# Preparing q and k for two attention heads at once, with DMAs that assemble each head's operands

## Chip, cores and metric

The kernel runs on one core of one Trainium2 chip. The metric is the device time of one execution in microseconds. A profiled execution has a span (first to last instruction) and a time of its own beside it.

## What is computed

Three stages, all on one core in one launch. Only the first is changed.

```
bits     = (x @ proj > 0) for x = q and x = k      # 6 bits a row: the bucket
mask     = q_bucket == k_bucket                     # per (batch, head)
scores   = where(mask, q @ k.T / 8, -1e9)           # 768 x 768
attn     = softmax(scores);  out = attn @ v         # 2 batches x 8 heads, head_dim 64
x        = out as (1536, 512)
y        = relu(x @ w_in)**2 @ w_out                # 512 -> 2048 -> 512
routed layer: tokens given to 8 experts by capacity, relu(y @ w1[e]) @ w2[e]
```

All values are fp32. A row of queries with no key in its bucket attends to all keys alike; this is the "fallback", made from the sum of v.

## The kernel before

`attention` handles the 16 heads one after another. TensorE, VectorE, ScalarE, GpSimd and SP (which issues the DMAs) each have a program written out in order, and they meet at semaphores. Four double PSUM banks are used: `PREP`, `ST`, `SM`, `O`. Tiles with a suffix 0 or 1 alternate by head (`i`, and `o = 1 - i` for the next head, `m = n + 1`).

While head `n` is attended to, head `n + 1` is prepared. Per head:

- `load` brings k and q (192 KB each, L148, L149), `load_v` brings v (L152), beside a half of ones in `v_raw`, so that one matmul yields numerators on 64 partitions and denominators on the other 64.
- `twice` on GpSimd (L194, L195) writes each row of q and k twice side by side; `transpose` (L476, `t_k`, `t_q`) turns them by six matmuls of 128 columns each, which gives both copies of the head on the two halves of the partitions.
- `k_high`, `q_high` (L256, L263) round to fp32r, `k_low`, `q_low` (L378, L383) subtract for the residual, `k_again`, `q_again` copy the high part again to where the scores need it. A high and a low part stand in the two halves of `ka` and `qa`, `qb`.
- `z_k`, `z_q` (L494, L495) project onto `proj`, with four matmuls of 384 columns each; `k_bits`, `q_bits` on VectorE and ScalarE turn signs into rows of 0, +-1 and 2^33 that stand below the high parts, so that a pair with unlike bits gets a hugely negative score from the same matmul.
- `scores` (L528) makes the scores row by row (two matmuls of 384 columns, six times), only for the row maxima, `row_max` (L400). `max_done`, then `rows` on TensorE (L537, L538) and ScalarE (L279, L280) bring the maxima and the sum of v into the operands of the next head (`qb`, `vsh`, and `vsl` for the residual, `v_low`, L414).
- `scores_t` (L515, L516) makes the transposed scores into the single bank `ST` (four matmuls of 384 columns, six times), `expo` (L285) the exponentials, `fallback` (L548) four matmuls, `weighted` (L552) multiplies with v: 12 calls of 384 columns in fp32, each two records in the profile.
- `numerator` (L421), `denominator` (L291), `invert` (L427: four reciprocals of 192 elements), `divide` and `low` on GpSimd (L212, L218) and `high` (L297) finish the head on its own 64 partitions, during the next one.

The order on TensorE of the steps of one head is written out by hand in `head` (L557). The last head's division is left to the beginning of `first_layer`. `load_weights` (L1389 to L1391) loads 8 MB for that stage once v of head 15 is issued; `first_layer` waits for it on `w_ready`. Between the stages all engines meet.

Of the kernel before, what the change touches and what calls it, by code (L numbers as in the profile page):

```python
# [6 lines left out]
BITS = 6  # L7
HEADS = B * NH
P = 128
# [3 lines left out]
PAIRS = HEADS // 2  # L13
TOK = B * S
# [15 lines left out]
FROW = D  # L30
MROW = 96
KF = MROW + 2
# [37 lines left out]
def attention(nc, banks, ident, finish, xt_hi, xt_lo, load_weights, q, k, v, proj):  # L70

    with ExitStack() as ctx:
# [3 lines left out]
        def sem(name):  # L82
            return ctx.enter_context(nc.semaphore("att_" + name))

        num, den, rden, xo = finish
        identr = sb("identr", [P, P], f32r)
        proj_sb = sb("proj_sb", [P, BITS])
        p_hh = sb("proj_hh", [P, P], f32r)
        p_ll = sb("proj_ll", [P, P], f32r)
        p_hl = sb("proj_hl", [P, P], f32r)  # L90
        p_h0 = sb("proj_h0", [P, P], f32r)
        off_q = sb("off_q", [P, 1])
        off_k = sb("off_k", [P, 1])
        guard = sb("guard", [P, 1])
        q_raw = [sb(f"q_raw{i}", [P, TT, D]) for i in range(2)]
        k_raw = [sb(f"k_raw{i}", [P, TT, D]) for i in range(2)]
        q_dup = sb("q_dup", [P, TT, 2, D])
        k_dup = sb("k_dup", [P, TT, 2, D])
        v_raw = [sb(f"v_raw{i}", [P, TT, P]) for i in range(2)]
        qa = [sb(f"qa{i}", [P, S], f32r) for i in range(2)]  # L100
        qb = [sb(f"qb{i}", [P, S], f32r) for i in range(2)]
        qc = [sb(f"qc{i}", [P, S], f32r) for i in range(2)]
        ka = [sb(f"ka{i}", [P, S], f32r) for i in range(2)]
        kb = [sb(f"kb{i}", [P, S], f32r) for i in range(2)]
        kg = sb("k_bits", [P, S])
# [3 lines left out]
        mn = sb("mn", [P, TT, KF], f32r)  # L109
# [3 lines left out]
        sel = sb("sel", [P, KF])  # L113
        vsh = [sb(f"vsh{i}", [P, P], f32r) for i in range(2)]
        vsl = [sb(f"vsl{i}", [P, P], f32r) for i in range(2)]
        PREP, ST, SM, O = banks

        names = ("zeroed", "made", "proj_in", "proj_split", "dup", "pool_steps", "tq", "tk", "zq", "zk", "st", "sm", "pv",
                 "mr", "qa_", "ka_", "qc_", "kc_", "qcs", "kbs", "ex", "mrc", "den_", "num_", "rec", "nrm", "xh", "xl",
                 "qlow", "klow", "fq", "fk", "mxs", "mns", "vslow", "vsum", "qk_in0", "qk_in1", "v_in0", "v_in1")  # L120
        (zeroed, made, proj_in, proj_split, dup, pool_steps, tq, tk, zq, zk, st, sm, pv,
         mr, qa_, ka_, qc_, kc_, qcs, kbs, ex, mrc, den_, num_, rec, nrm, xh, xl,
         qlow, klow, fq, fk, mxs, mns, vslow, vsum, qk_in0, qk_in1, v_in0, v_in1) = (sem(n) for n in names)
        qk_in, v_in = (qk_in0, qk_in1), (v_in0, v_in1)
# [5 lines left out]
        LOW, HIGH, BITROWS, TAIL = slice(0, D), slice(D, P), slice(FROW, FROW + FEAT), slice(MROW, KF)  # L130
# [7 lines left out]


        block = ctx.enter_context(nc.Block())  # L140

        @block.sync
        def _(sp):
            sp.dma_start(proj_sb[0:D, :], proj).then_inc(proj_in, 16)
            sp.dma_start(proj_sb[D:P, :], proj).then_inc(proj_in, 16)

            def load(n, i):
                sp.dma_start(k_raw[i][:], k_v[n]).then_inc(qk_in[i], 16)  # L148
                sp.dma_start(q_raw[i][:], q_v[n]).then_inc(qk_in[i], 16)  # L149

            def load_v(n, i):
                sp.dma_start(v_raw[i][:, :, VSL[i]], v_v[n]).then_inc(v_in[i], 16)  # L152
            load(0, 0)
            load(1, 1)
# [12 lines left out]
        @block.gpsimd  # L167
        def _(pool):
            pool.memset(ident[:], 0.0)
            pool.memset(sel[:], 0.0)  # L170
            pool.memset(off_q[:], 1.0)
            pool.memset(off_k[:], 1.0)
            pool.memset(guard[:], GUARD)
            pool.drain()
            pool.affine_select(out=ident[:], in_=ident[:], compare_op=ALU.not_equal, fill=1.0, base=0,
                               pattern=[[-1, P]], channel_multiplier=1)
            pool.memset(sel[:, KF - 1:KF], 1.0)
            pool.affine_select(out=off_q[:], in_=off_q[:], compare_op=ALU.is_ge, fill=0.0, base=-(FROW + BITS),
                               pattern=[[0, 1]], channel_multiplier=1)
            pool.affine_select(out=off_k[:], in_=off_k[:], compare_op=ALU.is_ge, fill=0.0, base=FROW + BITS - 1,  # L180
                               pattern=[[0, 1]], channel_multiplier=-1)
            pool.drain().then_inc(made, 1)

            def twice(m, i, count):

                pool.drain()
                pool.wait_ge(qk_in[i], count)
                if past(m, 1):  # L190
                    pool.wait_ge(tk, m)
                    pool.wait_ge(tq, m)
                pool.sem_inc(pool_steps, 1)
                pool.tensor_copy(k_dup[:], k_raw[i][:].unsqueeze(2).broadcast_to([P, TT, 2, D]))  # L194
                pool.tensor_copy(q_dup[:], q_raw[i][:].unsqueeze(2).broadcast_to([P, TT, 2, D])).then_inc(dup, 1)  # L195

            def sum_v(m, i, count):

                pool.drain()
                pool.wait_ge(v_in[i], count)  # L200
                if past(m, 1):
# [7 lines left out]
            def divide(n, i):  # L209
                pool.drain()  # L210
                pool.wait_ge(rec, n + 1)
                pool.tensor_tensor(xo[i][VSL[i], :], num[VSL[i], :], rden[VSL[i], :], ALU.mult).then_inc(nrm, 1)  # L212

            def low(n, i, pair):

                pool.drain()
                pool.wait_ge(xh, n + 1)
                pool.tensor_tensor(xt_lo[VSL[i], bass.ds(pair * S, S)], xo[i][VSL[i], :],  # L218
                                   xt_hi[VSL[i], bass.ds(pair * S, S)].bitcast(fp32), ALU.subtract).then_inc(xl, 1)

            sum_v(0, 0, 16)
            twice(1, 1, 32)
            sum_v(1, 1, 16)
            twice(2, 0, 64)
            with pool.Fori(1, PAIRS - 1) as it:
                for i in range(2):
                    n = 2 * it + i
                    sum_v(n, i, 16 * it + 16)
                    twice(n + 1, 1 - i, 32 * it + 32 * (i + 1))
                    divide(n - 2, i)  # L230
                    low(n - 2, i, it - 1)
            for i in range(2):
                n = HEADS - 2 + i
                sum_v(n, i, 16 * PAIRS)
                if i == 0:
# [1182 lines left out]
```

## Time and profile before

| | us |
|---|---|
| median of three runs | 900.96 (895.12 to 906.37) |
| the profiled execution's own time | 900.74 |
| its span | 899.0 |
| TensorE busy | 836.4 |
| VectorE busy | 478.2 |
| ScalarE busy | 387.4 |
| GpSimd busy | 317.7 |
| mean granted clock of TensorE | 0.961 of full |

Attention lasts until about 333 us of the span, the first layer until about 627, the experts until the end. Engines are PE (TensorE; PEld is its loading of weights), DVE (VectorE), ACT (ScalarE), POOL (GpSimd) and SP. A busy TensorE contains the pipeline's length, so the time that a matmul holds the engine is read from the starts of two neighbours. `x6` is a count of instructions merged in a row of the timeline.

### The profile page before, as it was taken

How to read it: one execution, taken by the hardware profiler on the slowest of the kernel's cores; microseconds unless marked ns; L12 is line 12 of the kernel's file. 1: busy time of each engine (PE TensorE's matmuls, PEld its weight loads, DVE VectorE, ACT ScalarE, POOL GpSimd, SP SyncE). 2: the span in 40 equal slices, each digit the busy share in tenths (PEclk: the TensorE clock that was granted, in tenths of full speed). 3: DMA queues.
4: the chain of work that ended last, by engine and by line, in shares of the span. 5: the costliest groups of instructions: out<-in, count | busy, mean ns of one | idle time of the engine just before them, and what ended most of it. 6: DMA issues, size and time to landing. Idle time of an engine off the chain costs nothing. (4 is left out here: it accounts for less than half of the span.)

```text
span 899.0 us, 14531 instructions
## 1 busy us (share of the span) xinstructions
PE 836.4 (93%) x4848; PEld 727.5 (81%) x4848; DVE 478.2 (53%) x954; ACT 387.4 (43%) x664; POOL 317.7 (35%) x299
## 2 busy tenths in 40 slices
PE   4999999999999979999999999997389998999996
PEld 2777777777777758889999999996279998999986
DVE  7688888878888846323224223423634553455410
ACT  3566656566665545454555455452011221112211
POOL 2134334333434337655565567562010100110111
PEclk8899999999999999999999999998569998999998
DMA  2011000011000630000000000000135453635361
GB/s 70 1 45 35 26 26 26 26 29 49 26 26 26 257 126 1 0 0 36 1 0 35 0 0 36 0 0 36 69 137 205 148 188 112 219 133 204 120 215 35
DMA packets 36656, 61.26 MB, mean 68 GB/s; under 512 B 14608, under 2 KB 18704, under 8 KB 36112
## 3 DMA queue, kind: packets, MB, share of 16 engines
q1 hardware_dynamic: 34576, 54.55, 17.8%
q0 software_dynamic: 2048, 6.29, 2.2%
q8 instruction: 19, 0.31, 0.1%
q14 instruction: 13, 0.11, 0.0%
HBM read 54.55 MB, written 6.29 MB: 68 GB/s over the span
## 5 line engine op out<-in xcount | busy, mean ns | idle before, releaser
L552 PE MATMUL banks<-pt,v_raw 128*128 128x384 f32 x384 | 149.2, 485 | 0.0
L821 DVE TENSOR_TENSOR h<-relu 128x384 f32<-128x384 f32 x64 | 42.1, 658 | 175.2 <-ACT relu L774 175.1
L682 POOL TENSOR_TENSOR wi_lo<-w_in_sb,wi_hi 128x512 fp32r<-128x512 f32 x64 | 84.2, 1317 | 96.7 <-ACT wi_hi L761 95.7
L1337 PE MATMUL banks<-x_cols,w_in_sb 128*128 128x192 f32 x512 | 96.8, 342 | 1.2 <-ACT x_cols L1121 1.1
L285 ACT ACTIVATE pt<-banks 128x768 f32<-128x768 f32 x96 | 77.9, 811 | 44.9 <-PE banks L516 44.0
L400 DVE TENSOR_REDUCE mx<-banks 128x1 f32<-128x768 f32 x96 | 89.7, 955 | 10.5 <-PE banks L528 6.3
L1351 PE MATMUL banks<-expert_hidden,w_out_sb 128*128 128x192 f32 x512 | 94.9, 336 | 0.0
L897 PE MATMUL banks<-xt_hi,wi_hi 128*128 128x384 f32 (+1 forms) x256 | 87.7, 342 | 3.5 <-POOL wi_lo L682 3.5
L688 POOL TENSOR_TENSOR wo_lo<-w_out_sb,wo_hi 128x512 fp32r<-128x512 f32 x64 | 83.7, 1308 | 14.1 <-ACT wo_hi L768 14.1
L1337 PEld LDWEIGHTS banks<-x_cols,w_in_sb 128*128 128x128 f32 x512 | 85.4, 197 | 3.7 <-issue 2.1
L897 PE MATMUL banks<-xt_lo,wi_hi 128*128 128x384 f32 (+1 forms) x256 | 87.2, 341 | 0.0
L897 PE MATMUL banks<-xt_hi,wi_lo 128*128 128x384 f32 (+1 forms) x256 | 87.1, 340 | 0.0
L1351 PEld LDWEIGHTS banks<-expert_hidden,w_out_sb 128*128 128x128 f32 x512 | 84.2, 194 | 0.8
L427 DVE RECIPROCAL rden<-den 64x192 f32<-64x192 f32 x60 | 78.2, 1325 | 0.7
L552 PEld LDWEIGHTS banks<-pt,v_raw 128*128 128x128 f32 x384 | 69.5, 189 | 9.9 <-ACT pt L285 0.2
L908 PE MATMUL banks<-wo_hi,h_hi 128*128 128x512 f32 x192 | 75.9, 395 | 1.4 <-DVE h_lo L824 1.3
L908 PE MATMUL banks<-wo_hi,h_lo 128*128 128x512 f32 x192 | 75.9, 395 | 0.0
L908 PE MATMUL banks<-wo_lo,h_hi 128*128 128x512 f32 x192 | 75.7, 394 | 0.0
L515 PE MATMUL banks<-qa,ka 128*128 128x384 f32 x192 | 72.0, 375 | 1.6 <-ACT vsh L280 0.4
L528 PE MATMUL banks<-kb,qc 98*128 98x384 f32 x192 | 69.7, 446 | 2.7 <-ACT qc L274 2.0
L774 ACT ACTIVATE relu<-banks 128x384 f32<-128x384 f32 x64 | 31.5, 493 | 92.0 <-PE banks L897 92.0
L516 PE MATMUL banks<-qb,kb 98*128 98x384 f32 x192 | 65.5, 341 | 0.0
(188 smaller groups left out, 1471.8 us busy)
## 6 DMA issues: line engine op xcount, KB each, us to landing
w_in_sb<-in_moe_w SPq DMA_DIRECT2D x8, 2048.0 KB, 9.4
w_out_sb<-in_moe_w SPq DMA_DIRECT2D x8, 2048.0 KB, 8.2
w_in_sb<-in_moe_w_in SPq DMA_DIRECT2D x1, 4096.0 KB, 13.4
w_out_sb<-in_moe_w_out SPq DMA_DIRECT2D x1, 4096.0 KB, 22.9
k_raw<-in_k SPq DMA_DIRECT2D x16, 192.0 KB, 2.7
q_raw<-in_q SPq DMA_DIRECT2D x16, 192.0 KB, 2.9
v_raw<-in_v SPq DMA_DIRECT2D x16, 192.0 KB, 2.8
y_rows<-y_rows_sb SPq DMA_DIRECT2D x4, 768.0 KB, 3.5
```

The lines of the kernel that those rows point to most:

```text
L285: act.activation(halves(pt[j % 2]), both(ST), ACT.Exp, scale=SCALE).then_inc(ex, 1)
L400: dve.tensor_reduce(mx[:, j:j + 1], both((PREP, SM)[j % 2]), AX.XY, ALU.max).then_inc(mxs, 1)
L427: dve.reciprocal(rden[VSL[i], c], den[VSL[i], c])
L515: pe.matmul(ST[:, h, 0:HALF], ka[i][:, kc], qa[i][:, c], start=True, stop=False)
L528: last = pe.matmul(slot[:, h, 0:HALF], qc[i][0:KF, qcol], kb[i][0:KF, h * HALF:(h + 1) * HALF], start=True, stop=True)
L552: last = pe.matmul(O[:, h, 0:HALF], v_raw[i][:, j, :], pt[j % 2][:, h * HALF:(h + 1) * HALF], start=False, stop=j == 5)
L682: pool.tensor_tensor(wil[i][:], wi[:].rearrange("p (k f) -> p k f", k=DT)[:, :, bass.ds(f * P, P)], wih[i][:].bitcast(fp32), ALU.subtract) ...
L688: pool.tensor_tensor(wol[i][:], wo[:, bass.ds(f * DM, DM)], woh[i][:].bitcast(fp32), ALU.subtract).then_inc(wols, 1)
L897: last = pe.matmul(PB[i][:, 0:HALF], w_[:, k, :], x_[:, xs], start=n == 0, stop=n == 3 * DT - 1)
L908: last = pe.matmul(PB[2 + t][:], h_[:, tc], w_[:], start=start and n == 0, stop=stop and n == 2, skip_group_check=True)
L1337: last = pe.matmul(PB[2 + f % 2][:, 0:CAP], w1s[i][:, k, f * P:(f + 1) * P], xgt[:, k, :], start=k == 0, stop=k == DT - 1)
L1351: last = pe.matmul(PB[4 + d % 2][:, 0:CAP], w2s[i][:, f, d * P:(d + 1) * P], hs[:, f, :], start=f == 0, stop=f == F2T - 1)
```

## The change

Heads are prepared in pairs. q and k of both heads are loaded side by side, transposed, split and projected once for the pair; `kh`, `kl`, `qh`, `ql` and the bit tiles hold head 0 of the pair on partitions 0 to 63 and head 1 on 64 to 127. Eight DMAs for each head (`assemble`), SBUF to SBUF, put its operands together: six of 64 partitions x 768 (192 KB) and two of 12 partitions. They replace `twice`, `k_again`, `q_again` and ScalarE's steps of the bits. All preparation lies in the even head of a pair; the scores of the next head, for the maxima, are made in each head, but in the odd one without preparation and so earlier.

Further parts:

- The fallback takes one weight tile `vs`, whose three rows carry the high and low parts, and two matmuls in place of four.
- The projection takes the three terms high x high, low x high, high x low: six matmuls of 384 columns for the pair for each of q and k.
- Division is for two heads at once, 128 partitions. Since it joins an odd head with the even one after it, the heads go in the sequence `ORDER` (9, 0, 1, ..., 8), `BLOCKS` says which block of `xt` each division fills, and the rows of `w_in` are loaded with their halves exchanged, in two DMAs of 64 partitions. The last division in `first_layer` is again that of one head; the last full one ends in the attention stage.
- To save memory `k_raw`, `q_raw` and the bit tiles lie in the tile of `w_out` (`spare`), so `load_weights` waits for the last assembly.
- Exponentials no longer start after an extra count, and each head's last `weighted` is placed behind the first `scores_t` of the next one.

```diff
-            with sp.Fori(1, PAIRS) as it:
-                for i in range(2):
-                    n = 2 * it + i
-                    sp.wait_ge(dup, n - 1)
-                    load(n, i)
-                    sp.wait_ge(pv, 6 * (n - 1) + 2)
-                    load_v(n, i)
+            def assemble(m, i):
+                mine, feat = VSL[i], slice(i * D + FROW, i * D + FROW + FEAT)
+                if m > 1:
+                    sp.wait_ge(st, 6 * (m - 1))
+                if i == 0:
+                    sp.wait_ge(kbits, m // 2 + 1)
+                sp.dma_start(kb[i][HIGH, :].bitcast(fp32), kh[mine, :].bitcast(fp32)).then_inc(k_set[i], 16)
+                sp.dma_start(kb[i][FEATURES, :].bitcast(fp32), kbit[feat, :]).then_inc(k_set[i], 16)
+                if i == 0:
+                    sp.wait_ge(qbits, m // 2 + 1)
+                sp.dma_start(qb[i][HIGH, :].bitcast(fp32), qh[mine, :].bitcast(fp32)).then_inc(q_set[i], 16)
+                sp.dma_start(qb[i][FEATURES, :].bitcast(fp32), qbit[feat, :]).then_inc(q_set[i], 16)
+                sp.dma_start(ka[i][LOW, :].bitcast(fp32), kl[mine, :].bitcast(fp32)).then_inc(k_set[i], 16)
+                sp.dma_start(ka[i][HIGH, :].bitcast(fp32), kh[mine, :].bitcast(fp32)).then_inc(k_set[i], 16)
+                sp.dma_start(qa[i][LOW, :].bitcast(fp32), qh[mine, :].bitcast(fp32)).then_inc(q_set[i], 16)
+                sp.dma_start(qa[i][HIGH, :].bitcast(fp32), ql[mine, :].bitcast(fp32)).then_inc(q_set[i], 16)
...
+            load_qk(1)
+            sp.wait_ge(cleared, 2)
+            assemble(0, 0)
+            assemble(1, 1)
+            for n in range(HEADS):
+                if n and n + 1 < HEADS:
+                    assemble(n + 1, 1 - n % 2)
+                    load_v(n + 1, 1 - n % 2)
+                if n % 2 == 0 and n // 2 + 2 < PAIRS:
+                    load_qk(n // 2 + 2)
+            sp.wait_ge(k_set[1], 64 * PAIRS)
+            sp.wait_ge(q_set[1], 64 * PAIRS)
             load_weights(sp)
...
+            def free_row(n, i):
+                pool.wait_ge(st, 6 * n + 6)
+                pool.memset(qb[i][0:1, :].bitcast(fp32), 0.0).then_inc(row_free, 1)
...
+            for n in range(HEADS):
+                i, p = n % 2, n // 2
+                expo(n, 0)
+                if n:
+                    denominator(n - 1, 1 - i)
+                expo(n, 1)
+                if i == 0 and p + 1 < PAIRS:
+                    k_high(p + 1)
+                    q_high(p + 1)
+                expo(n, 2)
+                if i == 0 and p:
+                    high(p - 1)
...
+            denominator(HEADS - 1, 1)
+            high(PAIRS - 1)
...
+            def even(n, p, prepare):
+                nxt = p + 1 if prepare else None
+                if past(n, 1):
+                    weighted(n - 1, 1, 5, 0)
+                scores_t(n, 0, 0)
+                if past(n, 1):
+                    weighted(n - 1, 1, 5, 1)
+                scores_t(n, 0, 1)
+                if prepare:
+                    t_k(p + 1)
+                fallback(n, 0)
+                if prepare:
+                    t_q(p + 1)
+                weighted(n, 0, 0, 0)
+                weighted(n, 0, 0, 1)
+                if prepare:
+                    z_k(p + 1)
+                scores_t(n, 0, 2)
+                if prepare:
+                    z_q(p + 1)
+                weighted(n, 0, 1, 0)
+                weighted(n, 0, 1, 1)
+                scores(n + 1, 1, p, 0, nxt)
...
+                rows(n + 1)
+
+            def odd(n, p, nxt):
+                weighted(n - 1, 0, 5, 0)
+                scores_t(n, 1, 0)
+                weighted(n - 1, 0, 5, 1)
                 if nxt:
-                    t_k(m)
-                scores_t(n, i, 0)
+                    scores(n + 1, 0, p + 1, 0, None)
+                scores_t(n, 1, 1)
+                fallback(n, 1)
+                weighted(n, 1, 0, 0)
```

On GpSimd each head has `free_row(n - 1)`, `sum_v(n + 1)`, and `low` (even) or `divide` (odd) behind them; after head 15 comes `low(PAIRS - 1)`. VectorE's odd head puts `invert` between the maxima, with its last two parts behind `max_done`.

## Rows read from the trace of the kernel before

**Rows 1.** Stretches: us, busy PE, PEld, DVE, ACT, POOL (counts), PEclk, DMA share, GB/s.

```profile
40.00:80.00 40.00, 39.04 (x191) 30.16 (x190) 33.49 (x40) 24.56 (x33) 14.30 (x14) 1.00 0.11 30
```

**Rows 2.** Timeline: the first scores, the first `scores_t` of heads 0, 14, 15.

```profile
14.98 0.96 PE L528 MATMUL banks<-kb,qc 98*128 98x384 f32 x4 [1.98 <-ACT qc L274]
...
25.13 0.68 PE L515 MATMUL banks<-qa,ka 128*128 128x384 f32 x1
...
298.59 0.44 PE L515 MATMUL banks<-qa,ka 128*128 128x384 f32 x1
...
318.25 0.45 PE L515 MATMUL banks<-qa,ka 128*128 128x384 f32 x1 [0.41 <-ACT vsh L280]
```

**Rows 3.** Timeline of heads 14 and 15, TensorE and ScalarE.

```profile
299.23 0.75 PEld L476 LDWEIGHTS banks<-ident,q_dup 128*128 128x128 f32 x6
...
309.09 0.19 PEld L515 LDWEIGHTS banks<-qa,ka 128*128 128x128 f32 x1
...
309.80 0.37 PEld L552 LDWEIGHTS banks<-pt,v_raw 128*128 128x128 f32 x2
...
316.22 0.73 PE L537 MATMUL banks<-identr,mn 128*98 128x128 f32 x6 [0.75 <-DVEq L410]
...
317.24 0.80 ACT L279 ACTIVATE qb<-banks 2x768 fp32r<-2x768 f32 x1 [3.55 <-PE banks L538]
...
322.12 0.19 PEld L515 LDWEIGHTS banks<-qa,ka 128*128 128x128 f32 x1 [0.22 <-ACT pt L285]
...
324.11 0.19 PEld L515 LDWEIGHTS banks<-qa,ka 128*128 128x128 f32 x1 [0.22 <-ACT pt L285]
```

**Rows 4.** Groups by line and shape, 60 to 250 us: busy, mean ns, idle before.

```profile
L427 DVE RECIPROCAL rden<-den 64x192 f32<-64x192 f32 x40 | 52.3, 1327 | 0.5
L400 DVE TENSOR_REDUCE mx<-banks 128x1 f32<-128x768 f32 x56 | 52.3, 956 | 3.4 <-issue 1.0 <-PE banks L528 0.8
L285 ACT ACTIVATE pt<-banks 128x768 f32<-128x768 f32 x59 | 47.9, 811 | 23.2 <-PE banks L516 22.7
...
L218 POOL TENSOR_TENSOR xt_lo<-x_out,xt_hi 64x768 f32 x10 | 18.3, 1826 | 11.7 <-ACT xt_hi L297 11.7
...
L256 ACT ACTIVATE ka<-banks 128x768 fp32r<-128x768 f32 x10 | 8.1, 814 | 0.2
...
L259 ACT ACTIVATE kb<-banks 64x768 fp32r<-64x768 f32 x10 | 8.0, 799 | 0.0
```

**Rows 5.** Timeline of SP: first and last of the three loads of weights.

```profile
298.97 0.48 SPq L1389 DMA_DIRECT2D w_in_sb<-in_moe_w_in  x1
...
300.05 14.23 SPq L1391 DMA_DIRECT2D w_gate_sb<-in_moe_w_gate  x1
```

**Rows 6.** View of the DMA issues: median us from issue to landing.

```profile
w_in_sb<-in_moe_w_in SPq DMA_DIRECT2D x1, 4096.0 KB, 13.4
...
q_raw<-in_q SPq DMA_DIRECT2D x16, 192.0 KB, 2.9
...
w_gate_sb<-in_moe_w_gate SPq DMA_DIRECT2D x1, 16.0 KB, 23.6
```

**Rows 7.** View of stretches at the start: first, highest and last of seven.

```profile
3.00:4.00 1.00, 0.00 (x0) 0.00 (x0) 0.48 (x5) 0.00 (x0) 0.00 (x0) 1.00 0.58 146
4.00:5.00 1.00, 0.00 (x0) 0.00 (x0) 0.79 (x6) 0.00 (x0) 0.00 (x0) 1.00 0.92 301
...
9.00:10.00 1.00, 0.96 (x5) 0.56 (x3) 0.43 (x1) 1.00 (x2) 0.71 (x3) 1.00 0.39 143
```

**Rows 8.** Timeline and stretches around an idle TensorE in the expert stage.

```profile
747.48 1.54 PE L1306 MATMUL banks<-ident,x_rows 96*128 96x96 f32 x8 [2.41 <-DMA x_rows<-y_rows,token_list]
...
747.00:748.00 1.00, 0.52 (x3) 0.53 (x4) 0.00 (x0) 0.00 (x0) 0.00 (x0) 0.65 0.00 0
...
754.00:755.00 1.00, 1.00 (x8) 0.98 (x8) 0.00 (x0) 0.11 (x1) 0.00 (x0) 0.94 0.77 295
```

**Rows 9.** Timeline: the last work of the attention stage.

```profile
331.80 0.89 ACT L291 ACTIVATE den<-banks,guard 64x768 f32<-64x768 f32 x1 [1.77 <-PE banks L552]
```

More of the change, by code:

```diff
@@ L155, in _ @@
+            load_qk(0)
+            for i in range(2):
+                sp.dma_start(proj_sb[VSL[i], :], proj).then_inc(proj_in, 16)
             sp.wait_ge(zeroed, 1)
@@ L221, in _ @@
[L221 to L235, printed above, removed]
-                    twice(n + 1, 1, 32 * PAIRS)
-                divide(n - 2, i)
-                low(n - 2, i, PAIRS - 2)
@@ new lines, in _ @@
+            k_high(0)
+            q_high(0)
+            rows(0, 0)
+            for n in range(HEADS):
+                i, p = n % 2, n // 2
[9 more added lines that the diff above has]
+                    high(p - 1)
+                expo(n, 3)
+                expo(n, 4)
+                expo(n, 5)
+                if n + 1 < HEADS:
+                    rows(n + 1, 1 - i)
@@ L429, in invert @@
                     dve.drain().then_inc(rec, 1)
-            def head(n, i, nxt, prev):
-                m, o = n + 1, 1 - i
-                if prev:
-                    numerator(n - 1, o)
+            def even(n, p, prepare):
+                if past(n, 1):
+                    numerator(n - 1, 1, p)
+                if prepare:
+                    k_low(p + 1)
+                    q_low(p + 1)
+                    k_bits(p + 1)
+                    q_bits(p + 1)
+                for j in range(6):
+                    row_max(n + 1, j)
+                max_done(n + 1)
+                v_low(n + 1, 1)
@@ L445, in head @@
                 if nxt:
-                    q_bits(m, o)
-                if prev:
-                    invert(n - 1, o, 2)
-                    invert(n - 1, o, 3)
-                if nxt:
-                    for j in range(6):
-                        row_max(m, o, j)
-                    max_done(m, o)
-                    if not past(m, 1):
-                        clear(1)
-                    v_low(m, o)
-            head(-1, 1, True, False)
-            head(0, 0, True, False)
-            head(1, 1, True, True)
@@ new lines, in _ @@
+            k_low(0)
+            q_low(0)
+            k_bits(0)
+            q_bits(0)
+            for j in range(6):
+                row_max(0, j)
+            max_done(0)
+            v_low(0, 0)
+            even(0, 0, True)
+            odd(1, 0, True)
+            with dve.Fori(1, PAIRS - 1) as p:
+                even(2 * p, p, True)
+                odd(2 * p + 1, p, True)
+            even(HEADS - 2, PAIRS - 1, False)
+            odd(HEADS - 1, PAIRS - 1, False)
+            numerator(HEADS - 1, 1, PAIRS)
@@ L597, in head @@
-                if nxt:
-                    rows(m, o)
-                weighted(n, i, 5, 1)
+                    scores(n + 1, 0, p + 1, 5, None)
+                weighted(n, 1, 3, 0)
+                weighted(n, 1, 3, 1)
+                scores_t(n, 1, 5)
+                weighted(n, 1, 4, 0)
+                weighted(n, 1, 4, 1)
+                if nxt:
+                    rows(n + 1)
             t_k(0)
@@ L603, in _ @@
             pe.wait_ge(proj_split, 1)
-            z_k(0, 0)
-            z_q(0, 0)
+            z_k(0)
+            z_q(0)
             for j in range(6):
-                scores(0, 0, j)
-            rows(0, 0)
-            with pe.Fori(0, PAIRS - 1) as it:
-                head(2 * it, 0, True)
-                head(2 * it + 1, 1, True)
-            head(HEADS - 2, 0, True)
-            head(HEADS - 1, 1, False)
+                scores(0, 0, 0, j, 0)
+            rows(0)
+            even(0, 0, True)
+            odd(1, 0, True)
+            with pe.Fori(1, PAIRS - 1) as p:
+                even(2 * p, p, True)
+                odd(2 * p + 1, p, True)
+            even(HEADS - 2, PAIRS - 1, False)
+            odd(HEADS - 1, PAIRS - 1, False)
+            weighted(HEADS - 1, 1, 5, 0)
+            weighted(HEADS - 1, 1, 5, 1)
 def routing_constants(nc, ctx):
@@ L885, in _ @@
         def _(pe):
[L886 removed]
+            pe.wait_ge(w_ready, 64)
             pe.sem_inc(rows_done, 2)
```

534 lines of the change are left out of this document (252 added, 282 removed).

## Prediction

> **What bounds the kernel now.** I read first the busy times by stretch [rows 1]: in the attention stage TensorE is busy 39 of every 40 us at full clock, VectorE 33.5, ScalarE 24.6, GpSimd 14.3. So a microsecond of TensorE work removed from a head is worth up to a microsecond, and work removed from the others is worth nothing by itself. Then the rhythm of the heads: the first score matmul of head 0 starts at 25.13, that of head 14 at 298.59, that of head 15 at 318.25 [rows 2]. Seven pairs take 273.5 us, 39.07 a pair, 19.5 a head.
>
> What TensorE pays comes from the starts, not from the durations (these contain the pipeline's length). One `scores_t`, four matmuls of 384 columns, holds it 0.71 us (309.09 to 309.80), 0.175 a matmul; a `scores_t` with both halves of `weighted` 1.99 (322.12 to 324.11), so half a `weighted` is 0.64; six transposes take 0.75 [rows 3]. I take 0.8 for `rows`, from six short matmuls (0.73) and the two of the last product beside them. One head before: 12 x 0.64 + 36 x 0.175 for both scores + 1.5 for the transposes + 8 x 0.175 for the projection + 4 x 0.175 for the fallback + 0.8 = 18.4. The rest, 1.1 to 1.2, is waiting: mostly 0.75 us before `rows`, where the row maxima end late [rows 3].
>
> **Work that goes from TensorE.** Per pair: 12 of 24 transposes (1.5 us), 4 of 16 projection matmuls (0.7; three terms for both heads replace two for each) and 4 of 8 fallback matmuls (0.7). 2.9 us a pair; busy work falls from 36.8 to 33.9.
>
> **Waits that come.** *At each head's start.* `rows` of the next head now ends a head, and `scores_t(n,0)` needs ScalarE's two copies of it. Those took 317.24 to 318.2, and the matmul came at 318.25, 1.2 us after `rows` had left TensorE [rows 2, 3]. Before, half a `weighted` and the transposes of k covered that; in the new order only half a `weighted` (0.64) does. Cost 0.55 a head. In the even head the second `scores_t` also waits for the exponential (0.81, [rows 4]): 0.3. There `rows` waits 0.2 for the maxima; in the odd head nothing, as the prefetched scores are earlier. Sum: 0.55 x 2 + 0.3 + 0.2 = 1.6 a pair.
>
> *For the assembly, in the odd head.* This is the step that decides. The scores of head n+1 now stand third in the odd head, and their first one needs all eight transfers of `assemble`. SP may issue these only when the last `scores_t` of head n-1 is done. Put zero at the start of the odd head; then SP starts at -2.0 (`rows` 0.8 and two halves of `weighted` 1.28 lie between, less the matmul's tail). TensorE arrives at the scores at 2.5: half a `weighted`, the 0.55 wait, `scores_t`, half a `weighted`. So the eight have 4.5 us. Behind the waiting matmul on TensorE stand `scores_t(n,1)`, the fallback and every `weighted` of the head: nothing can fill. No such transfer (64 rows of 3 KB, SBUF to SBUF) is in the trace, so I bound it. By issue: three issues in a row start 0.54 us apart [rows 5], the eighth at -2.0 + 7 x 0.54 = 1.8, and a 192 KB load lands after 2.9 at the median [rows 6], so 4.7; 4.4 if the way inside SBUF saves 0.3. By data: of the 2.9 about 2.0 are left when the bytes are taken off; eight loads of 192 KB at the start ran from 3 to 10 us, in seven rows from 146 to 143 GB/s with up to 301 between, some 1.57 MB in 6.4 us of it, or 0.8 us each [rows 7]. Six large transfers and two small: -2.0 + 2.0 + 4.8 + 0.2 = 5.0. I take 5.0, since bursts of equal size are the nearest rows: a wait of 2.5 us a pair. The lower end is 4.4 (1.9). The upper end is a rate half of the full one: 4 MB in 13.4 - 2.0 us [rows 6] is 368 GB/s, 0.53 us for 192 KB, doubled 1.07, and the last lands at 6.6 (4.1).
>
> A pair becomes 33.9 + 1.6 + 2.5 = 38.0 against 39.07: 1.1 x 7 = -7.7 us.
>
> **The clock.** After the copy of gathered rows TensorE was idle for 2.41 us up to 747.48, and the granted clock then stood at its lower level, 1.2 GHz, from 747 until it was back at 2.4 GHz in 754 [rows 8]: some 6.8 us at half speed, 3.4 us lost. The new wait of 2.5 us is as long, with 0.55 idle shortly before; the waits of before, 0.75 and 1.2 us, left the clock full [rows 1]. The fall at 747 shows that such a gap can do it, not that each does. I take four of seven: +13.6. Ends: none (the wait nearer 1.9), and seven, +24.
>
> **Other engines.** VectorE loses four of eight reciprocals a pair (1.33 us each; twice the partitions cost the same, as the copies to `ka` and `kb` show, 0.81 and 0.80 [rows 4]), two residuals and two bit steps; ScalarE the copies made twice; GpSimd the doubling copies. They were not the bound, and the new order keeps them off it: in the odd head VectorE has six maxima (0.96), four reciprocals, one copy, the tail of `max_done` and `v_low`, 13.2 of 18. `free_row` on GpSimd can stand behind `divide`, which ends some 2 us into the even head; its reader comes at 10. So nothing for these.
>
> **The start.** Before, the first scores came at 14.98 [rows 2], right after the last bit copy. Now the projection is loaded behind the four large loads and VectorE clears three large tiles before its first residual; on the other side the doubling copies go. I put q's bits at 15.4. Then six transfers: 15.4 + 2.0 + 5 x 0.8 + 0.1 = 21.5. All behind moves with it: +6.5 us (by issue alone 6.0, at half rate 8).
>
> **The end.** Head 14 has no preparation and no wait for its assembly: 15.1 + about 1.0 = 16.1 against 19.67 (298.59 to 318.25): -3.6. After head 15, the stage ended before with one copy of the denominators (331.80, [rows 9]), the last division being left to the next stage. Now `high` and `low` of the last full pair are queued behind it: 0.8 on ScalarE, 1.8 on GpSimd (`low` took 1.83 [rows 4]), +2.6, uncovered. The weights can't be loaded until the last assembly has left `wo`'s tile: issue at 5.5 us into head 14. They needed 24.7 us (298.97 issue, the last landed 23.6 after 300.05 [rows 5, 6]), so 30.2 against the stage's end at 16.1 + 18.2 = 34.3. Hidden by 4 us. `w_in` in two halves of 64 partitions hides too, unless these run at half rate.
>
> **Sum.** 899.0 - 7.7 + 13.6 + 6.5 - 3.6 + 2.6 = 910.4 span. The profiled execution took 900.74, 1.7 more than its span, and lies 0.2 below the median of 900.96. So 912.
>
> **Rivals.**
> 1. *A transfer that touches only half of the partitions runs at half rate* (slower; it decides once the last landing passes 6 us). Every assembly reads and writes 64 partitions. Wait 4.1: pair 39.6, 7 x 0.5 = +3.7; start +8; the weights 11.4 us later, 5 past the end after 1.6 us more of a late start, say +8; clock drops 6 x 3.4 = 20; -3.6 + 2.6. 899 + 38.7 + 1.7 = 939. For it: the equal bursts ran below the full rate. Against: the loads of the burst had small pieces that explain it. Halfway between this and my value lies 925. The Trainium skill's page "SBUF — State Buffer", section on the DMA port swizzle, states that partitions 0 to 63 reach only 8 of 16 ports and measured 196 GB/s at 1 MiB against 328 for all; no run here shows it yet. By its figure a transfer would take 1.0 us (an estimate from that page), and the time would be near 933.
> 2. *The wait is short and the clock stays* (landing at 4.4, no drop): 899 - 12 + 0 + 6 - 3.6 + 2.6 + 1.7 = 894. For it: the full rate needs only 3.2 us for the six. Against: no burst of this size in the trace ran at it.
> 3. *The assembly is hidden altogether* (the change does all it says): pairs of 33.9 + 1.6, so -25; 899 - 25 + 6 - 3.6 + 2.6 + 1.7 = 881. Against: SP alone needs until 1.8 to issue the eighth, and TensorE arrives at 2.5.
>
> **How the numbers follow.** Forecast 0.45 (905 to 919: two to six drops), rival 1 with its halfway case 0.33, rival 2 0.19, rival 3 0.03. The range reaches from rival 2 to past the halfway case, 893 to 933, leaving out rival 3 and the far part of rival 1. 2% (18 us) is about what a measurement of this kernel can tell from no change. Faster by more: rival 3, 0.03. Slower by more, over 919: rival 1 and the top of the forecast, 0.37. Within: 0.60.
>
> **What would show it.** TensorE idle of about 2.5 us once a pair ahead of the untransposed scores, ended by a DMA of the assembly; stretches of granted clock 0.5 in the attention stage, which had none after 27 us; the first scores at 21.5; a `low` alone after the last denominators; pairs of 38 us where the clock held. The prediction is wrong if transfers land within 4 us (then under 893), if the clock holds through the gaps (898), or if `w_ready` comes after the stage's end.

## The result and the profile after

| | before | after |
|---|---|---|
| median, us (4 runs each) | 899.62 (895.12 to 906.37) | 931.91 (929.66 to 934.47) |
| span of the profiled execution | 899.0 | 929.9 |
| TensorE busy | 836.4 | 827.0 |
| mean granted clock | 0.961 | 0.941 |

The ratio is 1.0353, with a 95% interval from 1.0281 to 1.0426: the change makes the kernel 3.5% slower. The forecast was 912 with a range of 893 to 933.

Page of the kernel after: busy time, with instructions behind the x.

```profile
PE 827.0 (89%) x4688; PEld 713.0 (77%) x4688; DVE 410.9 (44%) x882; ACT 321.7 (35%) x575; POOL 281.8 (30%) x283
```

VectorE lost 67 us of work and ScalarE 66, as the change means them to. Neither was the bound. The stretches answer to [rows 1]:

```profile
40.00:80.00 40.00, 35.61 (x157) 26.68 (x156) 23.62 (x30) 13.55 (x19) 5.32 (x7) 0.94 0.34 75
...
140.00:180.00 40.00, 35.52 (x157) 26.77 (x156) 23.54 (x28) 15.41 (x21) 8.86 (x11) 0.96 0.42 89
```

TensorE is now idle for 4.4 of 40 us where it was idle for one, and its mean clock is no longer 1.00. The view of TensorE's waits (line waited for: us in total, times, longest) names the place:

```profile
PE banks L523 <- issue: 34.1, 8, 8.1
...
PE banks L498 <- ACT v_sum_hi L282: 4.6, 16, 1.0
...
PE banks L498 <- ACT pt L288: 2.9, 9, 0.9
```

L523 is the matmul of `scores`. It waits eight times: once at the start (8.1) and once in each of seven odd heads. The profile names no releaser. In the program this matmul waits for `k_set` and `q_set`, which the eight DMAs of `assemble` count up, four each. The timeline of SP shows these for head 6:

```profile
138.25 0.51 SPq L158 DMA_DIRECT2D kb<-k_hi  x1
138.80 0.83 SPq L159 DMA_DIRECT2D kb<-w_out_sb  x1
...
142.88 0.60 SPq L167 DMA_DIRECT2D qa<-q_lo  x1
```

And TensorE's:

```profile
140.22 0.91 PE L546 MATMUL banks<-pt,v_raw 128*128 128x384 f32 x2
141.34 0.44 PE L498 MATMUL banks<-qa,ka 128*128 128x384 f32 x1 [0.20 <-ACT v_sum_hi L282]
...
146.69 0.71 PE L523 MATMUL banks<-kb,qb 128*128 128x384 f32 x2 [3.74 <-issue]
147.20 0.53 PE L498 MATMUL banks<-qa,ka 128*128 128x384 f32 x1
```

The odd head starts at 140.22. The first issue is 1.97 ahead of it, the eighth 2.66 behind it, and the scores start at 146.69, 6.47 behind it and 3.8 after the last issue. The L498 matmul behind them takes 0.53 where its like takes 0.34: the clock has fallen. Stretches of 1 us:

```profile
147.00:148.00 1.00, 1.00 (x5) 1.00 (x4) 0.56 (x1) 0.00 (x0) 0.69 (x1) 0.53 0.00 0
150.00:151.00 1.00, 1.00 (x4) 0.67 (x4) 0.02 (x1) 0.00 (x0) 0.00 (x0) 0.77 0.00 0
```

It stands at 1.2 GHz from 147.1 to 150.5, 3.4 us. Such a stretch comes with each of the seven waits; one stretch, at 102.7, is twice as long. Together they are 27.3 us at half speed. Some 2.6 us of this still fall inside the waits, where they cost nothing, so about 12.3 us are lost. The longest case, in which the scores start only at 104.21, shows the fall inside the wait:

```profile
102.00:103.00 1.00, 0.00 (x0) 0.00 (x0) 0.00 (x0) 0.00 (x0) 0.00 (x0) 0.84 0.99 215
```

In it TensorE does nothing, and the DMA engines are busy 0.99 of the time at 215 GB/s.

The start and head 14, to be read beside [rows 2]:

```profile
24.82 1.62 PE L523 MATMUL banks<-kb,qb 128*128 128x384 f32 x4 [8.13 <-issue]
...
34.82 0.69 PE L498 MATMUL banks<-qa,ka 128*128 128x384 f32 x1 [1.05 <-ACT v_sum_hi L282]
```

```profile
326.92 0.44 PE L498 MATMUL banks<-qa,ka 128*128 128x384 f32 x1 [0.20 <-ACT v_sum_hi L282]
```

(326.92 - 34.82) / 7 = 41.73 us a pair, against 39.07. The end, beside [rows 5, 9]: SP, then the other engines.

```profile
332.30 1.32 SPq L1419 DMA_DIRECT2D w_in_sb<-in_moe_w_in  x2
333.66 0.61 SPq L1420 DMA_DIRECT2D w_out_sb<-in_moe_w_out  x1
334.32 22.80 SPq L1421 DMA_DIRECT2D w_gate_sb<-in_moe_w_gate  x1
```

```profile
357.46 0.89 ACT L294 ACTIVATE den<-banks,guard 64x768 f32<-64x768 f32 x1 [1.77 <-PE banks L546]
358.38 0.84 ACT L299 ACTIVATE xt_hi<-x_out 128x768 fp32r<-128x768 f32 x1
366.55 1.15 ACT L789 ACTIVATE wi_hi<-w_in_sb 128x512 fp32r<-128x512 f32 x2 [7.33 <-DMA w_gate_sb<-in_moe_w_gate]
```

```profile
359.30 1.80 POOL L245 TENSOR_TENSOR xt_lo<-x_out,xt_hi 128x768 fp32r<-128x768 f32 x1 [6.74 <-ACT xt_hi L299]
...
368.65 0.69 PE L925 MATMUL banks<-xt_hi,wi_hi 128*128 128x384 f32 x1 [11.23 <-POOL wi_lo L710]
```

The attention stage ends at 361.1, and the first layer waits until 366.5 for weights issued at 332.3. The first layer's first matmul comes 7.5 us after the stage's end; before, it came 2.5 after (332.69 to 335.22).

**The whole difference.** Start +9.7 (34.82 against 25.13). Seven pairs +18.6, of which 12.6 is the clock (experiment 2). From head 14 to the end of the stage +0.1: 34.1 before [rows 2, 9], 34.2 now; the saving in heads 14 and 15 (2.7) pays for `high` and `low`. Weights +5.0. The rest of the program -2.5; of that, 1.7 is a clock drop in the expert stage that lasts 3.4 us in this profile, not 6.8 [rows 8]. Sum 30.9, which is 929.9 - 899.0.

### The profile page after: what moved, and what is told of

Its sections match the earlier page's. It is cut to its first block and busy times, and to the rows that moved or that the text cites. A ratio compares the mean times of both kernels' runs of the same rounds, so it can differ in the third digit from the quotient of the medians.

```text
span 929.9 us, 13830 instructions
## 1 busy us (share of the span) xinstructions
PE 827.0 (89%) x4688; PEld 713.0 (77%) x4688; DVE 410.9 (44%) x882; ACT 321.7 (35%) x575; POOL 281.8 (30%) x283
## 5 line engine op out<-in xcount | busy, mean ns | idle before, releaser
L546 PE MATMUL banks<-pt,v_raw 128*128 128x384 f32 x384 | 151.1, 498 | 0.0
L523 PE MATMUL banks<-kb,qb 128*128 128x384 f32 x192 | 73.4, 468 | 34.7 <-issue 34.1
L498 PE MATMUL banks<-qa,ka 128*128 128x384 f32 x192 | 78.1, 407 | 7.5 <-ACT v_sum_hi L282 4.6
L523 PEld LDWEIGHTS banks<-kb,qb 128*128 128x128 f32 x192 | 38.1, 207 | 58.5 <-issue 41.0
L499 PE MATMUL banks<-qb,kb 128*128 128x384 f32 x192 | 67.8, 353 | 0.0
```

The source lines that it names most:

```text
L498: pe.matmul(ST[:, h, 0:HALF], ka[i][:, kc], qa[i][:, c], start=True, stop=False)
L499: last = pe.matmul(ST[:, h, 0:HALF], kb[i][:, kc], qb[i][:, c], start=False, stop=True)
L523: last = pe.matmul(slot[:, h, 0:HALF], qb[i][:, qcol], kb[i][:, h * HALF:(h + 1) * HALF], start=True, stop=True)
L546: last = pe.matmul(O[:, h, 0:HALF], v_raw[i][:, j, :], pt[j % 2][:, h * HALF:(h + 1) * HALF], start=False, stop=j == 5)
```

## The experiments

Runs 1 to 4 have one baseline (the kernel before at a median of 896.49), 5 to 8 another (896.85), 9 to 11 a third (897.84). Scaled to the first, the changed kernel would take 1.0353 x 896.5 = 928. A pair is measured in all of them as the mean between the first assembly issued in an odd head and the last one, six pairs later: in the changed kernel (302.74 - 53.95) / 6 = 41.47.

**1. Only the four transfers that the scores read are waited for.** The last four fill `ka` and `qa`, which only `scores_t` of the next head reads. The wait for these goes there.

```diff
-                sp.dma_start(kb[i][HIGH, :].bitcast(fp32), kh[mine, :].bitcast(fp32)).then_inc(k_set[i], 16)
+                sp.dma_start(kb[i][HIGH, :].bitcast(fp32), kh[mine, :].bitcast(fp32)).then_inc(s_set[i], 16)
...
-            def scores_t(n, i, j):
+            def scores_t(n, i, j, p=None):
+                    pe.wait_ge(k_set[i], 32 * p + 32)
+                    pe.wait_ge(q_set[i], 32 * p + 32)
...
             def scores(m, i, p, j, prepared):
-                    pe.wait_ge(k_set[i], 64 * p + 64)
-                    pe.wait_ge(q_set[i], 64 * p + 64)
+                    pe.wait_ge(s_set[i], 64 * p + 64)
```

> One semaphore per head for the four transfers that the untransposed scores read (kb, qb and their bit rows), others for ka and qa, which only the transposed scores wait for. Theory (TensorE waits 3.7 us a pair for the last of eight landings, and the clock falls in that wait): the fourth landing comes about when TensorE arrives, the wait shrinks to under 0.8 us, no clock drop is left in the attention stage, pairs go from 41.7 to 36.5-37.5 us, the first scores come 3 to 5 us earlier, and the time is 885 to 900. Rival (the cost sits elsewhere, in GpSimd's, ScalarE's or TensorE's new order, and only shows at this wait): another wait of the same length appears at the next step and the time stays over 915.

Measured: 890.09 us, ratio 0.9924 (0.9888 to 0.9961); a repetition (11, last below) gave 890.21 and 0.9920. One semaphore more for each of the two sets of operand tiles turns a kernel that is 3.5% slower into one that is 0.8% faster than before. The timeline of an odd head that starts at 123.92, and a stretch:

```profile
125.84 0.81 PE L549 MATMUL banks<-pt,v_raw 128*128 128x384 f32 x2
126.49 0.61 PE L526 MATMUL banks<-kb,qb 128*128 128x384 f32 x2
126.94 0.40 PE L502 MATMUL banks<-qa,ka 128*128 128x384 f32 x1
```

```profile
120.00:160.00 40.00, 39.02 (x186) 28.47 (x184) 26.40 (x35) 16.58 (x23) 9.81 (x12) 1.00 0.45 97
```

The scores follow without a wait, the clock stays at 1.00, and a pair takes (266.72 - 49.41) / 6 = 36.22. The first scores start at 20.58, 2.5 us after the fourth issue (18.08). The 44.5 us between the two spans are the seven pairs (36.7, from the first `scores_t` of head 0 to that of head 14: 292.1 and 255.4), the start (4.2) and 3.6 behind the attention stage, which this edit doesn't touch and which differ in clock drops.

**2. The wait stays, and TensorE works in it.** Twenty matmuls into a free bank stand ahead of the wait.

```diff
             def scores(m, i, p, j, prepared):
+                    if prepared is None:
+                        pe.wait_ge(mxs, 6 * m - 1)
+                        for r in range(20):
+                            pe.matmul(PREP[:, r % 2, 0:HALF], p_hi[:], kh[:, 0:HALF], start=True, stop=True)
```

> Ahead of the wait for the assembly TensorE does 20 matmuls of 384 columns whose result is overwritten; nothing else changes, the wait still ends at the same landing. Theory that the clock is a cost of its own (seven stretches at the lower level, about 27 us, 1.95 us lost a pair): the drops after each wait vanish and the time falls by 11 to 15 us, to about 918. Rival (the clock costs nothing beyond the wait, or returns by itself): within 3 us of the changed kernel.

Measured: 916.39 us, ratio 1.0189 (1.0137 to 1.0241), 12 below the scaled 928.

```profile
138.11 3.94 PE L508 MATMUL banks<-k_hi,proj_hi 128*128 128x384 f32 x20
142.31 0.59 PE L527 MATMUL banks<-kb,qb 128*128 128x384 f32 x2 [0.27 <-issue]
142.74 0.34 PE L498 MATMUL banks<-qa,ka 128*128 128x384 f32 x1
```

The scores start as late as before, 6.47 after the head's start (135.84), but L498 takes 0.34: no clock drop in the heads, and a pair takes 39.67. The difference of 1.80 a pair, 12.6 in seven, is what the clock cost. So of the loss against experiment 1, a third is the clock and two thirds are the wait itself (39.67 - 36.22 = 3.45 a pair).

**3. The same bytes over all partitions.** The four transfers to `ka` and `qa` move 128 partitions x 384 columns, as many bytes as 64 x 768.

```diff
-                sp.dma_start(ka[i][LOW, :].bitcast(fp32), kl[mine, :].bitcast(fp32)).then_inc(k_set[i], 16)
-                sp.dma_start(ka[i][HIGH, :].bitcast(fp32), kh[mine, :].bitcast(fp32)).then_inc(k_set[i], 16)
+                sp.dma_start(ka[i][:, 0:HALF].bitcast(fp32), kl[:, 0:HALF].bitcast(fp32)).then_inc(k_set[i], 16)
+                sp.dma_start(ka[i][:, HALF:S].bitcast(fp32), kh[:, HALF:S].bitcast(fp32)).then_inc(k_set[i], 16)
```

> The four transfers into ka and qa move the same bytes as 128 partitions x 384 columns and not as 64 x 768, so ka and qa hold other values than they should. Theory that a transfer of 64 partitions runs at half rate (about 1.0 us for 192 KB): the last landing comes 0.7 to 1.9 us earlier, 2.9 us after its issue and not 3.8, and the wait falls from 3.7 to 1.8-3.0. Rival (issue and the fixed part of a landing alone set it): wait 3.7 as before, time unchanged within 2 us.

Measured, in two runs: 913.87 us, ratio 1.0164 (1.0087 to 1.0241).

```profile
137.13 0.61 SPq L167 DMA_DIRECT2D qa<-q_lo  x1
```

```profile
139.67 0.61 PE L523 MATMUL banks<-kb,qb 128*128 128x384 f32 x2 [2.49 <-issue]
...
216.16 0.61 PE L523 MATMUL banks<-kb,qb 128*128 128x384 f32 x2 [2.47 <-issue]
```

The stretch in which the wide transfers run:

```profile
137.00:139.00 2.00, 0.18 (x1) 0.00 (x0) 0.95 (x1) 1.28 (x2) 0.00 (x0) 1.00 0.86 297
```

It moves 297 GB/s at a DMA share of 0.86, where the changed kernel moved 215 at 0.99. The landing comes 2.5 us after the last issue in place of 3.8, and the wait is 2.49 in place of 3.74. Since the issues have the same pitch (4.65 us for the eight, 4.63 before), the 1.25 us are the data's. And 2.5 after the last issue is what experiment 1 had with four transfers: at this rate the issues set the landing, no longer the data. A pair takes 39.15. These waits are also of the length that the forecast assumed (2.42 to 2.51, and one of 2.88), and the clock fell with four of seven (at 60.7, 101.7, 217.8, 296.3): after 2.47 us of idling up to 216.16, but not after 2.49 up to 139.67. So at this length the wait alone does not tell whether the clock falls.

**4. All eight are waited for, but later.** In the odd head the scores move behind the third `scores_t` and the second `weighted`, and two of VectorE's reciprocals ahead of the maxima.

```diff
             def odd(n, p, nxt):
+                def ahead(j):
+                    if nxt:
+                        scores(n + 1, 0, p + 1, j, None)
...
                 scores_t(n, 1, 0)
                 weighted(n - 1, 0, 5, 1)
-                if nxt:
-                    scores(n + 1, 0, p + 1, 0, None)
                 scores_t(n, 1, 1)
...
                 weighted(n, 1, 1, 1)
-                if nxt:
-                    scores(n + 1, 0, p + 1, 3, None)
+                ahead(0)
                 scores_t(n, 1, 3)
```

> In the odd head the prefetched scores stand behind the third scores_t and its weighted, as in the even one, and VectorE does its first two reciprocals ahead of the maxima. The assembly is untouched. Theory: TensorE arrives at the scores 7.1 us into the head, after the landing at 6.45; no wait, no drop, pairs of 36 to 37 us; the start stays as it is; 888 to 900. Rival (the maxima then end too late): rows waits over 2 us a pair and the time stays over 905.

Measured: 897.17 us, ratio 0.9991 (0.9956 to 1.0025). A pair takes 36.43, only 0.2 more than in experiment 1, with no clock drop in the heads. So asking for fewer and asking later are two ways to the same cover. The 7 us between the two medians are the start (24.90 against 20.58: there nothing can be moved ahead), 1.5 for the pairs, and 1.3 left over.

**5. `w_in` is loaded during the heads.** Experiment 1, with `w_in` in eight pieces of 512 KB, one each in heads 3 to 10.

```diff
+                if 3 <= n <= 10:
+                    load_piece(sp, (n - 3) // 2, (n - 3) % 2)
```

> The split semaphores of the first experiment, and w_in in eight pieces of 64 partitions (512 KB each), one a head in heads 3 to 10, in place of two at the end; only w_out and the gate are loaded after the last assembly. Theory (the first layer waits for the weights: TensorE idle 11.1 us before it, of which some 7 are for them): that idle falls to 3.5-4.5 us, and the time by 6 to 8 us against 890, to 882-884. Rival (the pieces delay the assemblies by as much): waits of 1 us or more come back in the heads and nothing is won, 888 or more.

Measured: 885.60 us, ratio 0.9875 (0.9826 to 0.9925). The idle time ahead of the first layer's first matmul:

```profile
323.15 0.69 PE L931 MATMUL banks<-xt_hi,wi_hi 128*128 128x384 f32 x1 [6.17 <-POOL wi_lo L716]
```

It was 11.12 in experiment 1, so the wait for weights cost 5.0 us. I had expected less to be left, 3.5 to 4.5. What is left beyond the 3.46 of the kernel before is `high` and `low` of the last full pair, which no load touches; the expectation had left them out.

**6. `w_in` in one transfer.** Experiment 1 with one load of 128 partitions in place of two of 64.

> The split semaphores, and w_in in one transfer of 128 partitions, issued at the same place as the two halves, so that its rows are not exchanged and the first layer multiplies other rows. Theory of the half rate for 64 partitions: from the issue of w_in to the last weight takes 24 to 26 us and not 34, TensorE's idle before the first layer falls from 11.1 to 3.5-4.5 us, the time is 882-884. Rival (the weights were slow for their bytes beside assemblies, or for the later issue): still 32 us or more and 890.

Measured, in two runs: 886.31 us, ratio 0.9874 (0.9814 to 0.9935). The idle time ahead of the first layer is 6.17 again, the same 5 us less; 3.5 to 4.5 had been expected, with the same omission as in experiment 5, and 882 to 884 us. SP is held by the issue that stands behind the large ones:

```profile
293.60 13.69 SPq L1422 DMA_DIRECT2D w_gate_sb<-in_moe_w_gate  x1
```

It was held 22.8 us with halves. The same from the stretches: while the halves load in the changed kernel,

```profile
335.00:349.00 14.00, 13.49 (x60) 9.30 (x59) 9.20 (x14) 5.75 (x9) 1.98 (x3) 1.00 1.01 207
```

and while the one load runs here,

```profile
295.00:305.00 10.00, 9.80 (x47) 6.85 (x45) 5.85 (x10) 3.66 (x6) 2.29 (x2) 1.00 0.98 406
```

In both the 16 DMA engines are busy all the time (1.01 and 0.98 of it), and in one they move 207 GB/s, in the other 406. Rows of 8 KB are read in both. So the cut across the partitions halves the rate, and it shows as busy engines, not as idle ones.

**7. The fallback alone, in the kernel before.** One weight tile with three rows, two matmuls in place of four; nothing else of the change.

```diff
-                    for part, vs in enumerate((vsh[i], vsl[i])):
-                        pe.matmul(O[:, h, 0:HALF], vs[0:KF, :], qb[i][0:KF, c], start=part == 0, stop=False)
+                    pe.matmul(O[:, h, 0:HALF], vsl[i][0:KF, :], qb[i][0:KF, c], start=True, stop=False)
```

> The kernel before with only the fallback in one weight tile (three rows carry the sum of v as high and low part; two matmuls a head in place of four). Theory that TensorE's columns are what a head costs in the kernel before: 0.35 us a head, 5 to 6 us, ratio 0.994. Rival (waits at the exponential or the maxima take the gap): no change, ratio 1.000.

Measured: 897.32 us, ratio 0.9994 (0.9972 to 1.0017): nothing. The time went into a wait that was not there:

```profile
301.51 0.62 PE L552 MATMUL banks<-qb,vsl 99*128 99x384 f32 x2
302.58 0.44 PE L520 MATMUL banks<-qa,ka 128*128 128x384 f32 x1 [0.45 <-ACT pt L289]
```

The next `scores_t` needs the exponential that empties `ST`. In its view of waits for 40 to 290 us the first of these lines has 5.5 us in 13 heads, and the kernel before has no such line there. The second, the wait of `rows` for the maxima, was there before (5.0 us in 13 heads):

```profile
PE banks L520 <- ACT pt L289: 5.5, 13, 0.5
PE banks L542 <- DVEq L415: 5.1, 13, 0.4
```

0.42 a head takes back the 0.35 of two matmuls. TensorE's 39 of 40 us did not mean that each of its microseconds was on the path.

**8. All that helped, together.** Experiment 5, with `high` of the last full pair ahead of the last exponential and the projection loaded first.

```diff
-            load_qk(0)
             for i in range(2):
                 sp.dma_start(proj_sb[VSL[i], :], proj).then_inc(proj_in, 16)
+            load_qk(0)
...
+                if n == HEADS - 1:
+                    high(PAIRS - 1)
                 expo(n, 5)
...
-            high(PAIRS - 1)
```

> The fifth, and the last full pair's copy to xt_hi ahead of the last exponential in place of behind the last denominators, and proj loaded ahead of the first q and k. Theory: low of the last pair is hidden (2.7 us), the first k_low comes 2 us or more earlier, so the time is 4 to 5 us below the fifth, 877 to 880. Rival: the idle before the first layer is set by the weights alone, then only the start shows, 2 us.

Measured: 877.65 us, ratio 0.9806 (0.9752 to 0.9860), faster than both kernels. The idle time ahead of the first layer is back at 3.46, as before the change, and the first layer starts at full clock (0.34):

```profile
318.34 0.45 PE L932 MATMUL banks<-xt_hi,wi_hi 128*128 128x384 f32 x1 [3.46 <-POOL wi_lo L717]
318.63 0.34 PE L932 MATMUL banks<-xt_lo,wi_hi 128*128 128x384 f32 x1
```

The first scores start at 18.00, 3.4 sooner than in experiment 5.

**9. Which partitions?** Experiment 1 with `w_in` in three transfers: partitions 32 to 95 (2 MB), then 0 to 31 and 96 to 127.

```diff
-                for a in range(2):
-                    sp.dma_start(wi[(1 - a) * D:(2 - a) * D, :].rearrange("p (k f) -> p k f", k=DT), halves[a]).then_inc(w_ready, 16)
+                for c in (slice(32, 96), slice(0, 32), slice(96, P)):
+                    sp.dma_start(wi[c, :].rearrange("p (k f) -> p k f", k=DT), rows_of[c]).then_inc(w_ready, 16)
```

> Experiment 1 with w_in loaded in three transfers: partitions 32 to 95 first (2 MB), then 0 to 31 and 96 to 127 (1 MB each); the rows of w_in are not exchanged, so the first layer multiplies other rows than the reference, at the same cost. Two readings of the half rate. If it hangs on how many partitions a transfer touches, the first one moves the 207 to 211 GB/s that the halves 0 to 63 and 64 to 127 moved, the last weights come as late as in experiment 1 (SP held some 22.8 us, 11.1 us of idling ahead of the first layer), and the time is that of experiment 1, near 890. If it hangs on whether the partitions lie on one side of 64, the first moves some 400 GB/s, SP is held near 14 to 16 us, the idling falls to 6.2, and the time is near 886. I hold the second for likelier, 0.7.

Measured: 884.48 us, ratio 0.9883 (0.9807 to 0.9960). Stretches while the first transfer runs, and then the other two:

```profile
294.00:298.00 4.00, 4.00 (x19) 3.07 (x18) 3.12 (x5) 1.46 (x2) 2.03 (x2) 1.00 1.00 410
302.00:306.00 4.00, 3.49 (x14) 2.28 (x14) 2.01 (x3) 2.79 (x5) 0.00 (x0) 1.00 1.03 219
```

The first transfer landed 9.8 us after its issue, where the first half of experiment 1, with as many bytes, took 13.0.

The same 64 partitions' worth moves at 410 GB/s when it lies across partition 64, and at 207 when it lies on one side; 32 partitions on one side move 219. It is not the number of partitions. The Trainium skill's page "SBUF — State Buffer", in its section on the DMA port swizzle, has it so: 0 to 63 are 8 of 16 ports, 64 to 127 the other 8. By that a range from 32 to 95 has all 16, and the trace agrees. The whole load gains less than with one transfer (idling ahead of the first layer 7.33, SP held 18.1 us), since the two later parts go at the low rate. The expectation was 14 to 16 us and 6.2.

**10. The fallback's two matmuls issued twice**, in experiment 1.

```diff
-                    pe.matmul(O[:, h, 0:HALF], vs[i][:], qb[i][:, c], start=True, stop=False)
+                    for r in range(2):
+                        pe.matmul(O[:, h, 0:HALF], vs[i][:], qb[i][:, c], start=True, stop=r == 0)
```

> Experiment 1 with each of the two fallback matmuls of a head issued twice (the second starts the sum anew, so the result is the same): four matmuls of 384 columns in place of two, the number of the kernel before. If in the new order each of them holds the path, 0.35 us a head comes back, 5.6 in all: some 895 where experiment 1 has 890, and pairs of 36.9. If the wait for the exponential takes the gap there too, as it did in the kernel before, the time and the pairs of 36.2 stay. In experiment 1 the waits of scores_t for the exponential sum to 2.9 us in nine heads of 16, so I expect half and half: about 892 to 893.

Measured: 894.26 us, ratio 0.9969 (0.9937 to 1.0002), 4.1 above experiment 11, where the full price would be 5.6. A pair takes (273.67 - 52.14) / 6 = 36.92, 0.70 more than in experiment 1 and 0.57 more than in experiment 11, which is the same kernel as experiment 1: most or all of the two extra matmuls a head, not half of it, as I had expected. The waits for the exponential hardly shrank. From 40 to 290 us, first here and then in experiment 11:

```profile
PE banks L502 <- ACT pt L290: 1.5, 6, 0.3
...
PE banks L502 <- ACT pt L290: 1.8, 7, 0.3
```

So the same two matmuls are worth nothing in the order of before, and 0.25 (by the medians) to 0.35 us a head (by the pairs) in the order after.

**11. Experiment 1 again**, beside 9 and 10.

> Experiment 1 again, beside the two above on the same chip: ratio 0.992 to the kernel before, pairs of 36.2.

Measured: 890.21 us, ratio 0.9920 (0.9887 to 0.9953). In its profile a pair takes (267.46 - 49.34) / 6 = 36.35.

## Why the prediction was right or wrong

It had the sign and the mechanism, and it was 20 us low: 931.9 lies at the upper end of its range, and the kernel became 32 us slower where 11 was forecast. The mis-sized term is the landing of the assembly: of the 19.5 us between the two sums, 8.7 are the longer wait in the odd heads and 3.2 the start. Another 5.0 are the weights, at the same low rate.

| term | forecast | measured |
|---|---|---|
| pairs, without the clock | -7.7 | +6.0 |
| clock | +13.6 | +12.6 |
| start | +6.5 | +9.7 |
| head 14, `high` and `low` | -1.0 | +0.1 |
| weights | 0 | +5.0 |
| rest of the program | 0 | -2.5 |
| sum | +11.4 | +30.9 |

- **The wait in the odd head.** Right in place, cause and what stands behind it; TensorE arrived at 2.7 where 2.5 was forecast, and SP started at -2.0, as forecast. The failed step is "six large transfers and two small: -2.0 + 2.0 + 4.8 + 0.2 = 5.0. I take 5.0". It landed at 6.47, which is that step's own upper end, 6.6. I had taken the burst of equal loads as the nearest rows (0.8 us for 192 KB) and explained their low rate by small pieces. Those loads covered all 128 partitions, so they said nothing of this case, and why they were slow no run shows; experiments 3, 6 and 9 show half the rate for partitions on one side of 64. The price of half rate, 1.07 worked out from [rows 6], was close (192 KB at 207 GB/s are 0.95 us), and rival 1 was right as a mechanism. The wait was 3.74, not 2.5: 8.7 us in seven pairs.
- **The issue pitch** of 0.54 from [rows 5] was too short as well: eight issues took 4.63 from the first to the last, 0.66 each, since the two of 12 partitions take 0.83 and 0.78. So both ways of bounding the landing were too short: the issues alone, with 2.5 us behind the last one as in experiment 3, give 5.2, and the prediction had 4.4 to 4.7. The data come last, since experiment 3 takes 1.25 us from the 3.8 behind the last issue with the same issues.
- **The work of a pair.** Forecast 33.9 + 1.6 = 35.5; experiment 1, where the assembly costs nothing, has 36.2. The sum of starts was right within 0.7. Its term for the fallback, 0.7 a pair, holds or nearly holds in the new order (experiment 10: 0.57 to 0.70), though not in the old one (experiment 7): what a removed matmul is worth is a matter of what stands next to it, which a sum of durations does not show.
- **The clock.** The sum, 13.6 for 12.6, was nearly right by luck, through two errors that cancel: seven drops, not four, and each of 3.4 us, not 6.8 (one was). With waits nearly as long as I had taken them, experiment 3 had four of seven, which is luck as well, since the clock fell with some of these waits and not with others of the same length; with 3.7 us each wait brought one.
- **The start.** The same landing, and here mostly the issues: the bits came 0.5 later than forecast (15.92), the eighth issue was at 20.99, and even a landing 2.5 behind it would give 23.5, where 21.5 was forecast and 24.8 was measured.
- **The weights.** "Hidden by 4 us" failed by the rate again. I had seen that two halves would not hide at half rate, and had put that only into rival 1. From the first issue they needed 34.2 us (332.30 to 366.5) against 24.7 before. Experiments 5 and 6 take the 5 us away. The prediction had named `w_ready` behind the stage's end as a sign of being wrong, and so it came: 366.5 against 361.1.
- **The end.** `high` and `low` uncovered cost the 2.6 expected (2.75), and heads 14 and 15 together saved 2.7, not the 3.6 forecast for head 14. The 34.3 us that the prediction used from head 14 to the end don't fit its own terms (34.1 - 3.6 + 2.6 = 33.1); by these the weights would have been hidden by 3 us, not 4.
- **Rival 1** had 939 at full and 925 halfway; the measured time lies between. Its transfers were sized nearly right; it was too high in the clock (20 for 12.6) and in the weights (8 for 5), and too low in the start (8 for 9.7) and the pairs (3.7 for 6.0). The time worked out beside it from 1.0 us a transfer, near 933, was the closest of all. Rivals 2 and 3 fell for the changed kernel. Experiment 1 removes wait and clock drops with the same eight transfers: the trouble was that all eight were waited for.

## What to carry to other kernels

When one semaphore counts several transfers, ask of each reader which of them it reads: here four of eight, in the order of issue, were worth 38 us (928 to 890) with no transfer and no computation moved. Price a wait on the bound engine twice, by its own length and by the slower clock behind it: here 3.5 and 1.8 us a pair. Look at the DMA share only together with its GB/s, and let a transfer lie across partition 64, or cut it by columns: on one side of 64 the engines are just as busy at half the rate.

## What the runs showed of the hardware

- 64 partitions on one side of 64 moved 207 GB/s at a DMA share of 1.01; 64 partitions from 32 to 95 moved 410 at 1.00; all 128 moved 406 at 0.98.
- TensorE idled 2.42 to 2.51 us in six odd heads of experiment 3; the clock fell with three of these waits and not with the other three. It fell with the one of 2.88 us, and in the changed kernel with seven of seven waits of 3.65 to 3.75 us.
- The lower clock lasted 3.4 us in six of those seven cases and 6.8 in one.
- In the changed kernel the issue of a transfer of 12 partitions x 3 KB (36 KB) held SP for 0.78 to 0.93 us, one of 64 partitions x 3 KB (192 KB) for 0.47 to 0.89.
